# Scores of four tiles computed ahead, first block tile by tile with tokens as rows: one attention and two-block kernel

## What is computed

```python
scores = scale * np.matmul(q, k.transpose(0, 1, 3, 2))
kth = np.partition(scores, -top_k, axis=-1)[..., -top_k:-top_k + 1]
scores = np.where(scores >= kth, scores, -1000000000.0)
scores = scores - np.max(scores, axis=-1, keepdims=True)
attn = np.exp(scores)
attn = attn / (np.sum(attn, axis=-1, keepdims=True) + 1e-09)
attn_out = np.matmul(attn, v)
...
x = attn_out.transpose(0, 2, 1, 3).reshape(B * S, H * D)
h = x @ w_in                                       # 512 -> 2048
y = (np.maximum(h, 0.0) + alpha * np.minimum(h, 0.0)) @ w_out   # 2048 -> 512
out = ((y @ w_a) * (y @ w_b)) @ w_o                # 512 -> 1536 -> 512
```

## Time and profile before

| | us |
|---|---|
| three runs, median | 736.18 |
| lowest, highest | 733.26, 737.24 |
| the profiled execution | 734.61 |
| its span, first to last instruction | 732.8 |

### The profile page before, as it was taken

How to read it: one execution, slowest core, us unless ns; L and a number is a source line. 1 busy time by engine, 2 the same in 40 slices (tenths; PEclk the granted TensorE clock), 3 DMA queues, 4 the chain that set the end, 5 groups by cost and what they waited for, 6 DMA issues and landing times.

```text
span 732.8 us, 11682 instructions
## 1 busy us (share of the span) xinstructions
PE 639.7 (87%) x4592; PEld 556.5 (76%) x4592; DVE 424.7 (58%) x835; ACT 347.0 (47%) x622; POOL 308.8 (42%) x353
## 2 busy tenths in 40 slices
PE   3456779798799988999899968986999999999997
PEld 1344657586688876888678857876999999999996
DVE  5999969788879996999778002324533112211111
ACT  1666566657477766777747424433422212221111
POOL 0556876667576765766747636740000000000000
PEclk9886697959999999999989989998999999999999
DMA  9932121212122212221211310066001100010001
GB/s 324 382 137 76 39 76 42 73 39 76 53 76 78 76 41 103 77 62 54 75 48 38 125 77 1 0 238 222 0 1 44 44 0 1 1 44 0 1 1 43
DMA packets 28806, 52.92 MB, mean 72 GB/s; under 512 B 2768, under 2 KB 7376, under 8 KB 28752
## 3 DMA queue, kind: packets, MB, share of 16 engines
q1 hardware_dynamic: 28752, 52.19, 21.2%
HBM read 47.46 MB, written 4.72 MB: 71 GB/s over the span
## 4 chain that ended last, share of the span: by engine, by line
PE 66%; POOL 12%; DVE 8%; ACT 7%; issue 4%; DMA 2%; SPq 1%; ACTq 0%; POOLq 0%
PE ps L907 6%; PE ps L909 6%; PE ps L908 6%; PE ps L810 5%; PE ps L830 5%; PE ps L832 4%; PE ps L831 4%; DVE top L667 4%; PE ps L814 4%; PE ps L812 4%; DVE work L675 4%; PE ps L921 4%; PE ps L922 4%; PE ps L920 3%; POOL p_sb L392 3%
## 5 line engine op out<-in xcount | busy, mean ns | idle before, releaser
L667 DVE MAX8 top<-work 128x8 f32<-128x576 f32 x216 | 152.0, 745 | 0.0
L392 POOL TENSOR_TENSOR p_sb<-s_sb,p_sb 128x576 f32<-128x576 f32 x72 | 102.3, 1424 | 51.5 <-ACT p_sb L500 51.5
L810 PE MATMUL ps<-xT_parts,win_hi 128*128 128x256 f32 (+1 forms) x320 | 98.2, 307 | 12.1 <-POOL xT_parts L410 12.1
L675 DVE MATCH_REPLACE8 work<-top,work 128x576 f32<-128x576 f32 x144 | 105.8, 743 | 0.0
L706 DVE TENSOR_TENSOR ab<-ps,a_sb 128x384 f32<-128x384 f32 x36 | 20.1, 557 | 139.4 <-PE ps L909 132.9
L907 PE MATMUL ps<-y_parts,wab 128*128 128x384 f32 x288 | 97.4, 338 | 0.0
L909 PE MATMUL ps<-y_parts,wab 128*128 128x384 f32 x288 | 96.6, 336 | 0.0
L908 PE MATMUL ps<-y_parts,wab 128*128 128x384 f32 x288 | 96.6, 335 | 0.0
L812 PE MATMUL ps<-xT_parts,win_hi 128*128 128x256 f32 (+1 forms) x320 | 93.0, 291 | 0.0
L814 PE MATMUL ps<-xT_parts,win_lo 128*128 128x256 f32 (+1 forms) x320 | 92.9, 290 | 0.0
L830 PE MATMUL ps<-wout_hi,g_parts 128*128 128x512 f32 x144 | 65.3, 454 | 29.7 <-POOL g_parts L427 18.5
(11 more groups left out here) (76 smaller groups left out, 1400.4 us busy)
## 6 DMA issues: line engine op xcount, KB each, us to landing
k_sb<-in_kT SPq DMA_DIRECT2D x40, 288.0 KB, 3.2
v_sb<-in_v SPq DMA_DIRECT2D x36, 320.0 KB, 3.0
win_raw<-in_w_in SPq DMA_DIRECT2D x4, 1024.0 KB, 12.5
wout_raw<-in_w_out SPq DMA_DIRECT2D x4, 1024.0 KB, 12.9
wab_raw<-in_w_a SPq DMA_DIRECT2D x8, 384.0 KB, 5.3
wab_raw<-in_w_b SPq DMA_DIRECT2D x8, 384.0 KB, 5.7
wo_raw<-in_w_o SPq DMA_DIRECT2D x6, 512.0 KB, 6.3
q_sb<-in_qT SPq DMA_DIRECT2D x36, 64.0 KB, 3.1
```

The lines of the kernel that those rows point to most:

```text
L392: nc.gpsimd.tensor_tensor(p_sb[:, chain.par, c, :], s_sb[:, chain.slot, c, :], p_sb[:, chain.par, c, :], ALU.subtract).then_inc(masked, 1)
L667: largest = nc.vector.max(top32[:, pair.par, c, 8 * r:8 * r + 8], work[:, c, :] if r else s_sb[:, pair.slot, c, :])
L675: nc.vector.match_replace(work[:, c, :], top32[:, pair.par, c, 8 * r:8 * r + 8], work[:, c, :] if r else s_sb[:, pair.slot, c, :], -3.0e38)\
L810: nc.tensor.matmul(ps[:, bank, dst], win_hi[:, k, cols], xT_hi[:, k, 0:group.n], start=(k == 0), stop=False)
```

## The change

**Scores ahead.** The 16 pairs 20 to 35 (the last four tiles, `DIRECT` = 20, `KEPT` = 16) are scored in steps -2 to 4, three a step in -2 and -1 and two after, into a second set of PSUM banks as well as the first. ACT copies each from PSUM (`keep_scores`, 128x1152) to one of two slots, SP saves it to DRAM (`s_dram`), and from step 16 on loads it back into `s_sb`. Steps 17 on have no `score` and no `copy_scores`. k and v buffers shrink from three to two.

**First block tile by tile.** `up` has x as the stationary operand and w_in streaming, 512 columns: h has tokens as rows. A tile takes four steps ("quads" of 512 features), tile 0 too. alpha is a 128x2048 array (1 MB to load) and its product a TENSOR_TENSOR. g must be turned before `down`: four 128x128 transposes (`turn_g`) in the step after `up`, into PSUM bank 6, from where ACT makes two copies (`gT`, `g_hi`). `down` is as before. Steps 5 to 36 now do eight tiles; one is left behind the attention instead of two, and its `slope_and_sum` and `lo_of_g` are DVE's.

**Weights earlier.** The eight pieces of w_in are split in steps -1 to 4, those of w_out in steps 1 to 7: two pieces in each of steps -1 to 5, one in 6 and 7.

**Second block.** The same instructions; `ab` lies on `pos` instead of `ytok`, and the wait for the last `y_saved` is gone.

```diff
+AHEAD = {-2: [0, 1, 2], -1: [3, 4, 5], 0: [6, 7], 1: [8, 9], 2: [10, 11], 3: [12, 13], 4: [14, 15]}
+W_IN_AT = {-1: [0, 1], 0: [2, 3], 1: [4], 2: [5], 3: [6], 4: [7]}
+W_OUT_AT = {1: [5], 2: [6], 3: [7], 4: [0], 5: [1, 2], 6: [3], 7: [4]}
...
+            def save_scores(n):
+                sp.wait_ge(kept, n + 1)
+                sp.dma_start(s_dram[n], keep_sb[:, n % SLOTS, :]).then_inc(kept_saved[n % SLOTS], 16)
...
+            def slope_and_sum(seq):
+                q = seq % QUADS
+                pool.wait_ge(u_free, up_use(seq) + 1)
+                nc.gpsimd.tensor_tensor(neg[:, :], neg[:, :], alpha_sb[:, q * 512:(q + 1) * 512], ALU.mult)\
+                  .then_inc(slope_done, 1)
+                pool.wait_ge(slope_done, seq + 1)
+                nc.gpsimd.tensor_tensor(pos[:, :], pos[:, :], neg[:, :], ALU.subtract).then_inc(sum_done, 1)
...
+            def keep_scores(n):
+                _, buffer, _ = SCORE[DIRECT + n]
+                at = SC[buffer]
+                act.wait_ge(ahead, n + 1)
+                if n >= SLOTS:
+                    act.wait_ge(kept_saved[n % SLOTS], 16 * (n // SLOTS))
+                nc.scalar.activation(keep_sb[:, n % SLOTS, :], flat[:, at:at + 2 * S], ACT.Copy).then_inc(kept, 1)
...
+            def evict_x_turn(tile):
                 src = ps[:, U, :].rearrange("p (a n) -> p a n", a=DC)
+                act.wait_ge(u_full, turn_use(tile) + 1)
+                if tile:
+                    act.wait_ge(sum_done, QUADS * tile)
...
-            dve.wait_ge(y_saved[LAST], 16 * 2)
...
+            def up(seq):
+                tile, q = divmod(seq, QUADS)
+                cols = slice(q * 512, (q + 1) * 512)
...
+                    nc.tensor.matmul(ps[:, U, :], xT_hi[:, k, :], win_hi[:, k, cols], start=(k == 0), stop=False)
+                    nc.tensor.matmul(ps[:, U, :], xT_hi[:, k, :], win_lo[:, k, cols], start=False, stop=False)
+                    done = nc.tensor.matmul(ps[:, U, :], xT_lo[:, k, :], win_hi[:, k, cols],
                                             start=False, stop=(k == DC - 1))
...
+            def turn_g(seq):
+                pe.wait_ge(sum_done, seq + 1)
+                if seq:
+                    pe.wait_ge(ghi_done, seq)
+                for f in range(QUADS):
+                    done = nc.tensor.transpose(ps[:, GT, f * P:(f + 1) * P], pos[:, f * P:(f + 1) * P], ident[:, :])
+                done.then_inc(gt_full, 1)
...
+            for seq in range(LAST_UP, LAST_SEQ):
+                turn_g(seq)
+                up(seq + 1)
+                down(seq)
+            turn_g(LAST_SEQ)
```

More of the change, by code:

```diff
@@ L138, in attention_ffn @@
         copied = sem("copied")
+        ahead = sem("ahead")
+        kept = sem("kept")
         rank_step = sem("rank_step")
@@ L279, in save_y @@
-            def save_y(group):
-                for t in range(len(group.tiles)):
-                    sp.wait_ge(acc_out, group.tiles_before + t + 1)
-                    sp.dma_start(y_dram[group.row + t * P:group.row + (t + 1) * P, :], ytok[:, t, :])\
-                      .then_inc(y_saved[group.g], 16)
+                if what == "alpha":
+                    sp.dma_start(alpha_sb[:, :], alpha).then_inc(alpha_in, 16)
+                elif what.startswith("in"):
+                    sp.dma_start(win_raw[:, :, cols], w_in[:, cols].rearrange("(k p) n -> p k n", p=P))\
+                      .then_inc(win_in[n], 16)
+                else:
+                    sp.dma_start(wout_raw[:, 4 * n:4 * n + 4, :], w_out[cols, :].rearrange("(f p) n -> p f n", p=P))\
+                      .then_inc(wout_in[n], 16)
@@ L285, in load_w2, with save_y @@
+            def save_y(tile):
+                sp.wait_ge(acc_out, tile + 1)
+                sp.dma_start(y_dram[row(tile):row(tile) + P, :], ytok[:, :]).then_inc(y_saved[tile], 16)
             def load_w2(c):
@@ L459, in _ @@
                 step(i)
[L460 to L468 removed]
+            lo_of_g(LAST_UP)
+            lo_of_x(TILES - 1)
         @block.scalar
@@ L564, in step @@
-            def step(i):
-                score, chain, output, finished = pair(i + 3), pair(i + 1), pair(i), pair(i - 1)
-                up, down = fill(i)
-                opens = up is not None and up[1] == 0
+                act.wait_ge(u_full, turn_use(tile) + 1)
+                if tile:
+                    act.wait_ge(sum_done, QUADS * tile)
+                else:
+                    for slot in range(SLOTS):
+                        act.wait_ge(kept_saved[slot], 16 * KEPT // SLOTS)
+                nc.scalar.activation(xT_hi, src, ACT.Copy)
@@ L744, in score @@
                         done.then_inc(shared_bank, 1)
-                done.then_inc(scored, 1)
+                done.then_inc(scored if pair.kept is None else ahead, 1)
             def turn(pair, c):
@@ L833, in down @@
                                             start=False, stop=(f == FC1 - 1))
[L834 to L835 removed]
+                done.then_inc(down_done, 1)
             def step(i):
[L838 to L840 removed]
+                output, finished = pair(i), pair(i - 1)
+                ahead_now = AHEAD.get(i, [])
@@ L851, in step @@
-                if go_up is not None and not opens:
-                    up(*go_up, 1)
+                if direct(i) is not None:
+                    score(direct(i))
+                for n in ahead_now[:1]:
+                    score(pair(DIRECT + n))
+                if going_up(i) is not None:
+                    up(going_up(i))
                 if output is not None:
                     turn(output, 1)
-                if opens:
-                    up(*go_up, 0)
-                if go_down is not None:
-                    down(*go_down, 0)
@@ L859, in step @@
-                if opens:
-                    up(*go_up, 1)
-                if go_down is not None and go_down[0].n > P:
-                    down(*go_down, 1)
-                if first_turn(i) is not None:
-                    turn_x(first_turn(i), 0)
+                if going_down(i) is not None:
+                    down(going_down(i))
+                for n in ahead_now[1:]:
+                    score(pair(DIRECT + n))
+                if x_turn(i) is not None:
+                    turn_x(x_turn(i))
```

601 lines of the change are left out of this document (287 added, 314 removed).

## The result

| | before | after |
|---|---|---|
| median of 4 runs, us | 736.71 | 751.90 |
| lowest, highest | 733.26, 740.05 | 749.93, 755.15 |
| the profiled execution, its span | 734.61, 732.8 | 755.15, 752.1 |

The changed kernel takes 1.0211 times as long (95% interval 1.0149 to 1.0273): 15 us slower, and inside the range of 716 to 752 by only 0.1 us. The forecast was 735, no change, with a lean to faster. The profiled execution of the changed kernel was 3.3 us (0.4%) above its median, so differences of a few us between spans are read with that in mind.

What follows compares the result with a forecast made beforehand. DVE (36 pairs, 9.66 us apart) and PE were both taken to bound the attention without slack. Second block's start 492.3 + clock 7 + second block 233.0 = 732.3 us of span, given as 735; range 716 to 752.

Steps and rivals of the forecast that it cites:

- a lean to faster: Whole kernel: chance 0.40 of faster than 732.5 us, 0.28 within, 0.32 slower than 739.9.
- Steps 0 to 4: Early attention steps: two weight pieces and two more kept copies in each step's chain, 11.81 + 2.04 = 13.9 us.
- Step 4 to 5: From step 4's Relu to step 5's: 13.9 us like the steps before, putting the Relu of step 5 at 107.0.
- The save: Step -1: third kept copy waits for the first save to leave its slot; Relu of step 0 near 37.5, not 32.9.
- my upper end of 40: Relu of step 0: its late end, 40, if the queue is not ahead of the byte count.
- The clock: Steps 5 to 8: PE's pauses of 5 us and more bring half clock, 7 us in all, ends 0 and 25.
- the low clock lasts: Steps 5 to 8: each step at half clock adds 6 us; whole at 744 to 750, chance 0.25.
- The far rival: Steady steps: the 1.4 us pause drops PE's clock, each of 29 rounds adds 1.7 us; 784, chance 0.05.
- The second chain: Steps 6 to 36: `turn_g` waits for POOL's sum of the step before; rounds of 11.3 us with scores, 9.9 without.
- Tail and second block: After step 34's Relu: 65.0 us to the second block, which falls from 241.2 to 233.0 without the wait for `y_saved`.
- turn of x near 451: End of attention: sign that the turn of x comes near 451 us, with the second block near 499.

Runs made afterwards that it cites:

- Run 4: Changed kernel with ACT's high parts of the weights moved right behind the copy of the scores (except w_out's piece in step 4): 720.35 us.
- run 1: Also "the alpha run": changed kernel with SP asking for alpha in step 3 instead of step 5: 743.94 us.
- run 2: Changed kernel with w_in's second piece and the loads of v asked for behind the saves of step -1: 745.64 us.
- run 6: Also "the fillings": kernel of run 1 plus matmuls nobody reads on PE ending steps 5 to 7: 741.61 us, with longer fillings 738.96 us.
- run 3: Changed kernel with ACT's halves of h ahead of the eviction of the second turn in steps 5 to 36: 722.77 us.
- Run 10: Changed kernel with DVE's wait for the last rows of y in DRAM put back before the second block's first product: 759.08 us.
- Run 9: Changed kernel with edits of run 1, run 3 and Run 4, v's large load behind step -1's saves, loads ahead of saves from step 0: 674.86 us.
- run 8: Changed kernel without scores ahead, with the edits of run 1, run 3 and Run 4: 681.49 us.
- run 7: Changed kernel with the edits of run 1, run 2, run 3 and Run 4 together: 687.95 us.

## Why the forecast was wrong, and where it was right

- **Steps 0 to 4: part right.** 13.9 us a step were forecast, 14.2 measured; 1.2 us over four steps. ACT waits 0.28 us in each for the scores of its second kept pair, which PE makes with the granted clock at 0.50 to 0.84 from 40 to 100 us; the sum had full clock there. Run 4 shows more than the sum did: that chain was no necessity but an order. ACT's high parts stood behind everything, and POOL idled 4.4 us ahead of its low parts in each step.
- **Step 4 to 5: the step that failed.** The forecast gave it 13.9 like its neighbours. The load of alpha had been moved in SP's list, from the beginning to step 5, and grown from a small vector to 1 MB. My prediction walked every engine's list for the change but SP's. I named alpha's product on POOL as a cost, put its load at nothing, and never asked when alpha would be there or where POOL waits for it. It cost 9.0 us at R(5) and 2.8 more in step 5 through the clock in the profiled execution; between the medians run 1 took 8.0 us off. Where alpha is issued, and which waits stand ahead of it, could be read from the new code (`LOADS_AT` and SP's list). The Trainium skill, "DMA: Bandwidth & Descriptors", section "Anatomy of one DMA — SWDGE (gpsimd) path", says that "any semaphore wait happens on the issuing sequencer before dispatch". That section describes transfers that GpSimd issues; SP's row agrees with it here, for alpha was issued at 113.78, right behind the loads of k and q (112.93 and 113.31), which stand behind the same waits.
- **The save: right mechanism, wrong size.** I took the copy of step -1 to be held until R(0) came near 37.5, by counting bytes asked for before the fourth save. R(0) came at 41.9. The count went by the pace of before, 396 and 380 GB/s from 10 to 30 us; after the change the DMA engines moved 337 and 265 GB/s from 20 to 40. The term was 4.6 us and measured 8.8; run 2, with less ahead of the save, brought R(0) to 35.6. Even my upper end of 40 was short.
- **The clock: right mechanism, small in size.** 7 us were forecast. The steps 5 to 8 held 10.5 more than the count. By the Relus the alpha run took 4.0 of them away and the fillings, once they left almost no pause in two of three places, 4.0 more. Of the 2.6 that remain, 1.5 stand in step 6 and 1.0 in step 8, which opens a tile and whose next step is 1.0 shorter. The rival "the low clock lasts", with 744 to 750, came nearest by its number, but for another reason: alpha and the save make 13.4 of the 19.8 us between forecast span and span. That the result still fell into the range is luck, since the upper end of 752 stood for a clock that stays low.
- **The far rival fell.** With PE pausing 1.28 us before `turn_g` in each steady step, the granted clock was 1.00 in the stretch 221 to 399.4, above the 0.97 of before. The Trainium skill's rule on short idles between groups of matmuls ("TensorE: Matmul & The Clock Gate", section "A second HAM failure mode: psum-queue depth-cycling"), by which this rival would have been the forecast, at 784, is not borne out for a pause of this length once in 10 to 11 us.
- **The second chain: right.** `turn_g` waiting for the sum, 11.3 and 10.0 us a step where 11.3 and 9.9 were forecast; run 3 confirmed two of its members by taking them out, and corrected what would bind next.
- **Tail and second block: right**, 64.9 for 65.0 and 234.4 for 233.0. The parts fit too: the first `up` of the last tile began at 486.52, 14.3 us after step 36, and the last `down` waited 0.59 us where 0.8 were counted. The sign "turn of x near 451" does not follow from that sum, which gives 461; it came at 479.7, 18 to 19 us late like all behind the early steps. Run 10 confirmed the removed wait by putting it back. Of the 1.4 us in the second block 1.2 are PE's wait for the first product with w_o, which I had put at nothing.

The sum of the differences in span, forecast to profiled execution: save 4.4, steps 0 to 3 1.2, alpha 9.0, clock beyond the 7 us 3.5, steady steps and tail 0.4, second block 1.4: 19.9 of 19.8.

Why is the change slower, then, although its later parts gain 39 us? Because it puts three kinds of new work into the first eight steps (kept copies, weights at double pace, a first block that wants 1 MB of alpha) in an order in which they wait for each other. Run 9 shows the changed kernel 61 us below the kernel before once four places in two lists are put right; 53 of them come without kept scores too (run 8).

What stays open: the 8.8 us that run 9 still waits for saves were not removed; and the same kind of edits were not tried on the kernel before, so how much of the 61 us belongs to the change and how much to the order of the lists is not shown.

## What to carry to other kernels

When a load moves in a list, date its issue as you date an engine's work: find the waits ahead of it on the queue that issues it, and ask who stands still until it lands, and whether that engine waits for it sooner than it reads it. When two engines hand work back and forth, put what the other one waits for first in the list: an eviction of 0.6 us in the wrong place cost 29 us here, two copies of 1 us in the wrong place 32. And judge an idea such as keeping scores only when the queues around it are in order: it cost 3 to 5 and 6.5 us with two orders of the lists and earned 6.6 with the third.

## What was new about the hardware

Half clock shows after short pauses, and not always in the first instructions behind them. From `turn_g` to the second turn PE took 6.1 us behind every pause of up to 1.3 us (runs 3, 4, 6 and the changed kernel), 7.5 to 7.8 behind 2.24, 2.57, 2.59, 4.00 and 6.67 (runs 6 and 7), and 8.0 to 8.8 behind 4.7 to 9.3 (runs 1, 3, 4 and the changed kernel). The four transposes by themselves took 0.66 us at full clock and 1.11 at half, but 0.88, 0.80 and 0.66 behind 2.24, 2.57 and 2.59: there the clock fell during them or right behind them. And a save to DRAM is dated by what is asked for ahead of it: 3.1 us from issue to landing in the median, 11.0 behind 3 MB of loads.
